# Transposing q and k together in a fused attention and mixture-of-experts kernel, with a head's work in other slots

## What is computed

```python
def _attn_ref(q, k, v, centroids):
    B, H, S, D = q.shape            # 2, 8, 768, 64
    scale = 1.0 / np.sqrt(D)
    ...
    q_assign = np.argmax(np.einsum('bhsd,hcd->bhsc', q_n, c_n), axis=-1)
    k_assign = np.argmax(np.einsum('bhsd,hcd->bhsc', k_n, c_n), axis=-1)
    mask = q_assign[:, :, :, None] == k_assign[:, :, None, :]
    scores = scale * np.matmul(q, k.transpose(0, 1, 3, 2))
    scores = np.where(mask, scores, -1000000000.0)
    ...
    return np.matmul(attn, v)

x = _moe_ref(x=x, ...)              # 1536 tokens, 512 columns, 8 experts
return _moe2_ref(x=x, ...)
```

## Times and profile before

| what | us |
|---|---|
| median of 3 runs | 832.93 (832.70 to 833.83) |
| profiled execution, its time | 836.38 |
| profiled execution, its span | 834.6 |
| PE busy | 804.2 (96%) |
| DVE busy | 450.1 (54%) |
| ACT busy | 383.4 (46%) |
| POOL busy | 347.0 (42%) |
| one head in the middle, slot 0 to slot 0 | 17.31 (147.37 to 164.68) |
| attention, to its last value product | about 300 |

### The profile page before, as it was taken

One profiled execution on the slowest core, in us unless ns is written; L12 is line 12 of the kernel. 1 busy time (PEld: TensorE's weight loads), 2 busy tenths in 40 slices (PEclk: granted clock), 3 DMA queues, 4 the chain that ended last, 5 costly groups with the idle time before them and its releaser, 6 DMA issues.

```text
span 834.6 us, 13743 instructions
## 1 busy us (share of the span) xinstructions
PE 804.2 (96%) x4370; PEld 681.0 (82%) x4371; DVE 450.1 (54%) x795; ACT 383.4 (46%) x757; POOL 347.0 (42%) x343
## 2 busy tenths in 40 slices
PE   7999999999999948999999999999999999999995
PEld 4899999999999836888888888888888888888884
DVE  5688888888888875212212212335445444555452
ACT  3788888888888845222223223212223322332222
POOL 6436654354642118678857857766000100010001
PEclk9999999999999977999999999999999999999999
DMA  4344433324111147699859859665000100010001
GB/s 108 99 118 155 121 97 101 116 66 128 48 49 35 57 131 241 217 373 327 293 201 335 269 201 349 256 227 177 1 1 1 50 1 1 0 51 1 1 0 51
DMA packets 45428, 105.43 MB, mean 126 GB/s; under 512 B 5200, under 2 KB 12880, under 8 KB 44368
## 3 DMA queue, kind: packets, MB, share of 16 engines
q1 hardware_dynamic: 29584, 60.92, 22.1%
q0 software_dynamic: 15808, 44.04, 15.8%
HBM read 92.37 MB, written 6.29 MB: 118 GB/s over the span
## 4 chain that ended last, share of the span: by engine, by line
PE 93%; ACT 3%; DVE 2%; DMA 1%; issue 1%; POOL 0%; POOLq 0%; SPq 0%; DVEq 0%
PE ps L1468 16%; PE ps L1511 15%; PE ps L1435 13%; PE ps L1455 13%; PE ps L1256 7%; PE ps L1272 4%; PE ps L1242 4%; PE ps L1243 4%; PE ps L1270 4%; PE ps L1284 3%; PE ps L1196 2%; PE ps L1445 2%; PE ps L1216 2%; PE ps L1207 1%; PE ps L1177 1%; PE ps L1413 1%
## 5 line engine op out<-in xcount | busy, mean ns | idle before, releaser
L396 POOL TENSOR_TENSOR weights<-raw_w,weights 128x2048 fp32r<-128x2048 f32 x34 | 157.2, 4627 | 47.7 <-DMA weights<-in_moe_w 35.6
L1511 PE MATMUL ps<-weights,g_t 128*128 128x512 f32 x576 | 140.8, 394 | 0.8 <-DVE g_t L1122 0.8
L1468 PE MATMUL ps<-y_t,weights 128*128 128x512 f32 x576 | 139.6, 391 | 0.0
L1511 PEld LDWEIGHTS ps<-weights,g_t 128*128 128x128 f32 x576 | 107.3, 188 | 25.1 <-DVE g_t L1122 2.1
L1468 PEld LDWEIGHTS ps<-y_t,weights 128*128 128x128 f32 x576 | 108.1, 188 | 24.0 <-POOL weights L396 0.2
L1435 PE MATMUL ps<-weights,x_t 128*128 x456 | 112.2, 402 | 1.7 <-DVE x_t L1088 1.7
L927 DVE TENSOR_TENSOR p_t<-ps,p_t 128x384 fp32r<-128x384 f32 x192 | 98.9, 551 | 27.5 <-ACT p_t L629 27.1
L567 POOL DMA_INDIRECT out<-y_sb,order_u x12 | 11.8, 982 | 236.9 <-ACT y_sb L778 235.1
L1455 PE MATMUL ps<-weights,h_t 128*128 x456 | 109.4, 395 | 0.3 <-DVE h_t L1094 0.3
L1435 PEld LDWEIGHTS ps<-weights,x_t 128*128 128x128 f32 x456 | 85.9, 192 | 20.2 <-issue 2.3
L762 ACT ACTIVATE ps<-g_a,half 128x512 f32<-128x512 f32 x48 | 33.2, 692 | 145.9 <-DVE g_b L1117 145.9
(11 more groups left out here) (178 smaller groups left out, 1080.4 us busy)
## 6 DMA issues: line engine op xcount, KB each, us to landing
raw_w<-in_moe_w SPq DMA_DIRECT2D x32, 1024.0 KB, 6.4
weights<-in_moe_w POOLq DMA_DIRECT2D x28, 1024.0 KB, 9.2
qk_t<-qk_t SPq DMA_DIRECT2D x32, 192.0 KB, 2.6
raw_w<-in_moe_w_in SPq DMA_DIRECT2D x4, 1024.0 KB, 6.1
weights<-in_moe_w_in POOLq DMA_DIRECT2D x4, 1024.0 KB, 7.8
raw_w<-in_moe_w_out SPq DMA_DIRECT2D x4, 1024.0 KB, 7.4
weights<-in_moe_w_out POOLq DMA_DIRECT2D x4, 1024.0 KB, 11.7
raw<-in_q SPq DMA_DIRECT2D x16, 192.0 KB, 2.8
```

The lines of the kernel that those rows point to most:

```text
L396: pool.tensor_tensor(weights[:, unit % 2, 1, c * CHUNK:(c + 1) * CHUNK], low_chunk(unit, c), high_chunk(unit, c).bitcast(F32), ALU.subtrac ...
L1468: last = mm(ps[:, UP_BANKS[n % 2], :], wi[:, a, k, f * P:(f + 1) * P], y_ts[g % 2][:, b, k, :], start=(k == 0 and j == 0), stop=(k == KC - ...
L1511: last = mm(ps[:, t, :], g_t[:, n % 2, a, t * P:(t + 1) * P], wo[:, b, f, :], start=(f == 0 and j == 0), stop=(f == FC2 - 1 and j == 2))
```

## The change

q and k of a head are loaded side by side, so that a tile of `raw` is 128 rows by 64 columns of q and 64 of k. PE transposes `raw` itself, in two batches of three tiles; the transposed tile has q in partitions 0 to 63 and k in 64 to 127. ACT copies it whole into `whole` with a per-partition scale (1/8 for q, 1 for k). GpSimd makes the high part and the low part from `whole` straight into `qk_t` (for heads 0 and 1 ACT and DVE do it from PSUM). Four DMAs per head place the parts: the high queries to two places, the low queries, the low keys, the high keys. The centroids get low parts for both halves. In the slots: the first batch stands in slot 5 of the head before the one in which it stood, the second in slot 2; the cluster products and rows both in slot 4; the one-hots in slot 0; DVE copies both query one-hots, ACT both key one-hots. In slot 4 DVE divides after the subtractions, not before. The heads' loops cover one pair of heads less, and the last four heads are written out.

```diff
-BATCH_OF = {0: 0, 2: 1, 3: 2, 4: 3}
-FIRST_BANKS = ((4, 5, 6, 7), (4, 5, 6, 4))
+FIRST_BANKS = ((4, 5), (6, 4))
-WARM = (11, 11, 9)
+WARM = (7, 11, 9)
...
             def load_head(h, u):
                 if h >= 2:
-                    sp.wait_ge(halves_done, 2 * (h - 1))
-                sp.dma_start(raw[:, u, 0:QT, :], q_h[bass.ds(h, 1)].squeeze(0)).then_inc(qk_in[u], 16)
-                sp.dma_start(raw[:, u, QT:, :], k_h[bass.ds(h, 1)].squeeze(0)).then_inc(qk_in[u], 16)
+                    sp.wait_ge(tr_done, 2 * (h - 1))
+                sp.dma_start(raw[:, u, :, 0:D], q_h[bass.ds(h, 1)].squeeze(0)).then_inc(qk_in[u], 16)
+                sp.dma_start(raw[:, u, :, D:], k_h[bass.ds(h, 1)].squeeze(0)).then_inc(qk_in[u], 16)
...
-            def move_keys(h):
+            def place_halves(h):
                 u = h % 2
+                high = qk_t[:, u, B1:B1 + QT, :].bitcast(F32)
+                low = qk_t[:, u, B2:B2 + QT, :].bitcast(F32)
+                sp.wait_ge(high_done, 2 * (h + 1))
+                sp.dma_start(qk_t[0:D, u, A1:A1 + 2 * QT, :].bitcast(F32).rearrange("p (a t) n -> p a t n", a=2),
+                             high[0:D].unsqueeze(1).broadcast_to([D, 2, QT, P])).then_inc(q_high, 16)
+                sp.wait_ge(low_done, 2 * (h + 1))
+                sp.dma_start(qk_t[D:, u, A1:A1 + QT, :].bitcast(F32), low[0:D]).then_inc(q_low, 16)
                 sp.wait_ge(ct_done, h + 1)
-                sp.dma_start(qk_t[0:D, u, B2:B2 + QT, :].bitcast(F32), qk_t[D:, u, B1:B1 + QT, :].bitcast(F32)).then_inc(keys_low, 16)
-                sp.wait_ge(keys_low, 16 * (h + 1))
-                sp.dma_start(qk_t[D:, u, B1:B1 + QT, :].bitcast(F32), qk_t[0:D, u, B1:B1 + QT, :].bitcast(F32)).then_inc(keys_high, 16)
+                sp.wait_ge(q_low, 16 * (h + 1))
+                sp.dma_start(low[0:D], low[D:]).then_inc(k_low, 16)
+                sp.wait_ge(q_high, 16 * (h + 1))
+                sp.dma_start(high[0:D], high[D:]).then_inc(k_high, 16)
...
-            def split_operands(h, j, i, u, first):
...
+            def split_operands(h, b, u):
+                if b == 0:
+                    pool.wait_ge(s_done, QT * (h - 1))
+                pool.wait_ge(whole_done, 2 * (h - 2) + b + 1)
+                hi, lo = (qk_t[:, u, t + HALF * b:t + HALF * (b + 1), :].rearrange("p t n -> p (t n)") for t in (B1, B2))
+                pool.tensor_copy(hi, whole[:, b]).then_inc(high_done, 1)
+                pool.wait_ge(high_done, 2 * h + b + 1)
+                pool.tensor_tensor(lo, whole[:, b], hi.bitcast(F32), ALU.subtract).then_inc(low_done, 1)
...
-            def copy_queries(h, u):
-                pool.wait_ge(opa_done, 4 * h + 2)
-                pool.tensor_copy(qk_t[0:D, u, A2:A2 + QT, :], qk_t[0:D, u, A1:A1 + QT, :]).then_inc(b2_done, 1)
...
+            def first_high(h, b, bank):
+                act.wait_ge(tr_done, 2 * h + b + 1)
+                t = B1 + HALF * b
+                act.activation(qk_t[:, h, t:t + HALF, :].rearrange("p t n -> p (t n)"), x_bank[bank], ACT.Copy,
+                               scale=qscale[:, 0:1]).then_inc(high_done, 1)
+            def copy_whole(h, b, bank=7):
+                act.wait_ge(low_done, 2 * (h - 1) + b + 1)
+                act.wait_ge(tr_done, 2 * h + b + 1)
+                act.activation(whole[:, b], x_bank[bank], ACT.Copy, scale=qscale[:, 0:1]).then_inc(whole_done, 1)
+            def copy_key_onehots(h, u):
                 act.wait_ge(oh_tr, h + 1)
+                act.wait_ge(k_low, 16 * (h + 1))
...
             def attend(h, u, first, ahead):
...
-                    if s == 4:
-                        normalise(h, 0, ahead < 2, first)
+                    if s == 5 and ahead >= 2:
+                        highest_score(h + 2)
+                        best_clusters(h + 2)
...
+                    if s == 4:
+                        normalise(h, 0, ahead < 2, first)
...
+                    if s == 0 and ahead >= 1:
+                        copy_query_onehots(h + 1, 0, un)
...
             def scores(h, c, u, first):
                 if c == 0:
-                    pe.wait_ge(oh_done, 2 * (h + 1))
-                    pe.wait_ge(ohq_done, h + 1)
-                    pe.wait_ge(b2_done, h + 1)
-                    pe.wait_ge(keys_high, 16 * (h + 1))
+                    pe.wait_ge(oh_done, h + 1)
+                    pe.wait_ge(ohq_done, 2 * (h + 1))
+                    for moved in (q_high, q_low, k_low, k_high):
+                        pe.wait_ge(moved, 16 * (h + 1))
```

## The result

| | us |
|---|---|
| before, median of 5 runs | 833.58 (832.70 to 834.30) |
| after, median of 5 runs | 828.37 (828.01 to 830.00) |
| ratio, with its 95% interval | 0.9944 (0.9933 to 0.9954) |
| after, profiled execution: time, span | 828.37, 826.6 |

The kernel is 4.7 us faster by the ratio, 5.2 by the medians, where 9.7 was forecast. The page's first part of the kernel after, beside the earlier trace rows: PE has 100 instructions and 13 us less, POOL 18 less, DVE 8 more.

A forecast was written before the change was run, and what follows sets the result against it. PE's own instructions were taken to set a head's time in attention. The terms -9.9 - 4.0 + 2.2 + 1.4 + 0.6 gave -9.7 us off the median 832.93, so 823.2 us, with a range of 817 to 830.

The forecast's parts named there:

- point 5: Ahead of the first head: products and first scores start sooner, slot 0 of head 0 near 21 us; -4.0 us.
- point 2: Heads' slots: what PE waits for from DVE, ACT, GpSimd and DMAs keeps up after the change; no cost.
- point 3: Slot 1: one-hot transposes no longer cover ACT's o_t copy, so the back product starts later; 0.16 a head, +2.2 us.
- Point 4: Slots 3 and 4, eight heads: GpSimd's weight pieces hold up DVE's 128x6 addition and so the division; +1.4 us.
- Point 1: Heads' loop: half of PE's operand transposes go, 29 batches at 0.34 us each; -9.9 us.
- The walk of the slots: Slots 0 to 5 of a head after the change: lengths 2.41, 2.8, 2.41, 2.07, 4.2 and 2.41 us.
- rival B: Eight heads: the DVE and GpSimd port delay passes whole to PE, 7.7 instead of 1.4 us; 829.5 us, chance 0.06.
- rival C: The start gains nothing, as small runs delay first transposes and the DMAs queued behind them; 827 us, chance 0.05.
- Point 6: Slot 4 of heads 14 and 15: the division behind the subtractions has nothing to cover it; +0.6 us (0 to 1.2).

The follow-up runs named there:

- e8: Changed kernel with every operand batch of three transposes in the heads' loop done twice, same outcome; 834.95 us in its one run.
- e4: Changed kernel with the head loops of PE, ACT and DVE written out instead of looped; 825.24 us, ratio to before 0.9888.
- e3: Changed kernel with PE's three one-hot transposes of slot 0 put back behind the value product; 828.45 us, ratio to before 0.9928.
- e6: Changed kernel with DVE's division in slot 1 put ahead of the second query one-hot copy; 833.52 us, ratio to before 0.9998.
- e7: Changed kernel with the edits of e3 and e6 together; 829.99 us, ratio to before 0.9961.
- e1: Changed kernel with GpSimd's weight pieces moved from behind the splits to behind the cluster candidates; 833.35 us, ratio to before 0.9988.
- e2: Changed kernel with eight weight pieces of 256 columns instead of four of 512, same place; 824.93 us, ratio to before 0.9881.
- e10: Changed kernel with smaller pieces, heads written out, division first in heads 14 and 15, and head 0's high queries by 192 KB DMA plus GpSimd copy; 819.35 us, ratio 0.9829.
- e9: Changed kernel with q and k loaded one behind the other in 1536-byte runs, computing something else with the same instructions; 828.35 us, one run.
- e5: Changed kernel with division ahead of subtractions in heads 14 and 15, and gate loads issued behind head 0's placing DMAs; 829.31 us, ratio to before 0.9944.
- e0_before: The kernel before, unchanged, profiled a second time; 834.0 us, span 832.2.

## Why the gain was half of the forecast

The direction and the main mechanism held, and the time lies in the range, but the gain is half of the one forecast. Most of what is missing is the start (point 5): -4.5 was forecast with head 0, -1.2 came. The heads hit their sum only because a gain left out (point 2) and two costs left out or set too low (points 3 and 4) nearly cancel. Against the second profile of before (the sum's own terms in the same parts):

| part | forecast | measured |
|---|---|---|
| start and head 0 | -4.5 | -1.2 |
| heads 1 to 13 | -5.8 | -5.2 |
| heads 14 and 15 | +0.6 | +1.2 |
| rest | 0 | -0.4 |
| sum | -9.7 | -5.6 (spans), -5.2 (medians) |

**Point 1, the transposes: right.** A batch costs 0.32 to 0.33 (e8), 0.34 was taken.

**Point 2: right, and better than its sum.** None of GpSimd's, ACT's or the DMAs' lateness appeared. A clean head saves 0.95 (17.31 to 16.36), while the sum had two batches less point 3's cover, 0.52. The walk of the slots had it: its six lengths add up to 16.30, with the cover 16.46, since, by the slots' lengths, two short waits of before (the cluster rows' and one in slot 1) went with the batches. But the sum was made from batches alone, and was not held against the walk. For 13 heads that is -12.4 instead of the sum's -7.2: 5.2 us left out.

**Point 3, the o_t cover: the size near, the cause only half.** A clean slot 1 takes 3.01 to 3.08, 0.2 to 0.3 above the walk's 2.8, where 0.16 was forecast. Looped heads pay 0.2 more in slot 1 and 0.37 in all for being in a loop (e4), which the prediction had nowhere: +3.7 us for ten, by the two without pieces. That this bites after the change and hardly did before fits two chains that now end together in slot 1, o_t on ACT and one-hots with division on DVE; the fit is argued, the runs show only what each order gives. Putting one chain back changed nothing (e3), shortening the other alone made it worse (e6), and both together moved the wait to slot 2 (e7).

**Point 4, DVE against GpSimd: right mechanism, wrong size.** +1.4 was taken, halfway to nothing since it seemed open which starts first; it was 8 x 0.52 = +4.2 (e1, e2). In after the addition starts 0.07 to 0.08 us behind the piece in all eight heads and ends with it: the order repeats, head for head. Here rival B came true in part. The failed step is half of the price by the chance of who starts first (1.4 of the 2.8 us missing) and a head's cost of 0.35 that was 0.52 (the other 1.4); head 10 of before had the cost on show, 0.36 for an addition 0.80 late. The Trainium skill (SBUF — State Buffer, SBUF: two separate sides) says that the one that starts first holds the shared ports for its whole instruction. By that, the trace agrees for the addition: 1.24 us where the piece ran 1.27, 0.70 with half the piece, and 1.30 or 0.16 where the two start together (e4). The reciprocal behind it was not held (0.19, beside the second piece).

These three nearly cancel in heads 1 to 13: -5.2 left out on one side, +3.7 and +2.8 on the other, so -5.8 becomes -4.5. The traces have -4.6 and -5.2, of which 0.6 and 1.2 are what the heads of before took above 17.31 in the two executions. That the heads came out near the forecast is luck.

**Point 5, the start: the largest miss, and two steps failed.** First, the base: slot 0 of head 0 at 26.10 held some 1.2 us of a PE at half clock, which the prediction took for waiting that the change removes (5.1 us gained where first scores gained 2.5). The granted clock of that stretch would have told. Another 0.6 us was in the first scores of that execution alone (17.65, in the other 17.05). Second, the DMA: the low queries were given 2.5 us from issue to landing, near the median of the earlier trace rows. It took 4.2, behind one of 384 KB issued 0.7 us ahead (e10: 3.0 behind 192 KB; runs and gate loads ruled out by e9 and e5). With the products 0.4 later than forecast, that is the 2.2 us by which the first scores missed 15.1. It is rival C's outcome at the scores, by another cause. Head 0, for which 1 us was to be given back, gave none (16.81 us; 17.21 in e0_before).

**Point 6, the end: +1.2, the upper bound.** Shown by e5's (a).

**What is open.** Why PE's clock fell near 22 us in one of two executions of before (it fell there in e5_ends too, during a wait of 3.18 us); what in the loop costs the 0.37 us; whether DVE's amount of work is what bounds slots 1 and 2.

## What to carry to other kernels

An engine's saved work is a gain only up to the next chain: walk each slot as the longest of its chains, make the sum from that walk, and expect small costs that were hidden (a loop's own instructions, a copy's cover) to appear. Where two engines contend for a resource, take the full price if one starts clearly first, since with the schedule that order repeats (8 of 8 heads at 0.07 us); only a start within 0.02 us went both ways (6 and 2 of 8). See whether the longer instruction can be cut before moving it. Before a gap in a profile is counted as removable, read the granted clock of that stretch, and of a DMA in a chain read what was issued just ahead of it.

## What the hardware showed

- A VectorE addition of 128x6, 0.16 us alone, took up to 1.30 us beside a GpSimd subtraction of 128x512, and up to 0.70 beside one of 128x256 (in e2_pieces_small); a comparison of 128x192, 0.36 alone, up to 1.48. It ended 0.03 us behind the subtraction. Where both started within 0.02 us, it was held in six heads and passed in 0.16 in two.
- A head without pieces took 16.74 us in a loop and 16.37 written out, once VectorE had hardly any slack beside TensorE; in the kernel before, 17.31 and 17.27.
- A DMA of 192 KB within SBUF landed 4.2 us after its issue behind one of 384 KB issued 0.7 us ahead, 3.0 behind one of 192 KB. Loads of 192 KB in runs of 256 bytes landed after 3.25 and 3.65 us, in runs of 1536 after 2.48 and 2.51, which made no difference to this kernel's time.
- The same start of the same program ran at a granted clock of 0.52 over three microseconds in one execution and at 1.00 in another, with nearly equal waits just ahead of it.
